# First FFN product of an fp32 attention and FFN kernel computed by Strassen's seven block products, with weights streamed per batch

## The reference, cut to what matters

```python
attn = softmax(scale * q @ k.T + bias, masked) @ v         # 2 batches, 8 heads, 768 x 64; window of 96 keys + 8 global
x = attn laid out as [2, 768, 512]
h = x.transpose(0, 2, 1) @ U @ V;  u = x + h.transpose(0, 2, 1)
x = u + np.maximum(u @ w_ch1, 0.0) @ w_ch2                 # layer 1: 512 -> 2048 -> 512
mixed = real(fft over the 768 rows, then over the 512 columns of x);  u = x + mixed
un = (u - mean) / sqrt(var + 1e-6)
out = u + np.maximum(un @ w_ch1, 0.0) @ w_ch2              # layer 2, its own weights
```

## Time and profile before

| | us |
|---|---|
| median of 3 runs | 726.27 |
| lowest, highest | 722.5, 728.18 |
| profiled execution, its own time | 723.18 |
| its span in the trace | 721.4 |
| TensorE busy | 707.2 (98%) |
| VectorE, ScalarE, GpSimd busy | 268.1, 160.5, 122.4 |
| DMA | 37.09 MB, mean 51 GB/s |
| mean granted TensorE clock | 0.992 of full |

### The profile page before, as it was taken

How to read it: one execution, slowest core, us unless ns; L and a number is a source line. 1 busy time by engine, 2 the same in 40 slices (tenths; PEclk the granted TensorE clock), 3 DMA queues, 4 the chain that set the end, 5 groups by cost and what they waited for, 6 DMA issues and landing times.

```text
span 721.4 us, 9877 instructions
## 1 busy us (share of the span) xinstructions
PE 707.2 (98%) x3888; PEld 639.8 (89%) x3888; DVE 268.1 (37%) x671; ACT 160.5 (22%) x445; POOL 122.4 (17%) x77
## 2 busy tenths in 40 slices
PE   8899999999999999999999979999999999999998
PEld 6799999999999989999979869888999999989897
DVE  7466543453231221213526976245612121212212
ACT  4466543432111111111211212212211111111110
POOL 1633000000042482000002551000000850000000
PEclk9899999999999999999999999999999999999999
DMA  7663222000023131000000211000000310101011
GB/s 203 205 220 127 100 99 98 2 2 0 1 77 96 50 125 60 0 0 1 0 1 30 88 58 59 1 0 1 1 1 0 116 59 0 44 0 44 6 37 44
DMA packets 28499, 37.09 MB, mean 51 GB/s; under 512 B 2896, under 2 KB 19408, under 8 KB 28336
## 3 DMA queue, kind: packets, MB, share of 16 engines
q1 hardware_dynamic: 28464, 36.62, 15.6%
HBM read 36.61 MB, written 3.15 MB: 55 GB/s over the span
## 4 chain that ended last, share of the span: by engine, by line
PE 92%; DVE 5%; SPq 2%; DMA 1%; issue 0%; ACT 0%; DVEq 0%
PE hidP L609 12%; PE hidP L611 12%; PE yP L620 12%; PE yP L621 12%; PE yP L622 12%; PE hidP L610 12%; PE aP L545 4%; PE aP L519 4%; PE aP L532 2%; PE yP L545 1%; PE hidP L569 1%; PE yP L519 1%; DVE Y L1116 1%; DMA K<-k_win 1%; DVE UN L1133 1%; PE aP L653 1%
## 5 line engine op out<-in xcount | busy, mean ns | idle before, releaser
L1028 DVE SCALAR_TENSOR_TENSOR hidL<-hidP,hidH 128x384 fp32r<-128x384 f32 x128 | 71.2, 556 | 324.1 <-ACT hidH L795 324.1
L609 PE MATMUL hidP<-UTH,WH 128*128 (+1 forms) x512 | 173.8, 339 | 0.0
L611 PE MATMUL hidP<-UTH,WL 128*128 (+1 forms) x512 | 172.4, 337 | 0.0
L610 PE MATMUL hidP<-UTL,WH 128*128 (+1 forms) x512 | 171.8, 336 | 0.0
L620 PE MATMUL yP<-WH,hidH 128*128 128x512 f32 x384 | 152.2, 396 | 0.0
L795 ACT ACTIVATE hidH<-hidP 128x384 fp32r<-128x384 f32 x128 | 62.9, 491 | 401.5 <-PE hidP L611 401.5
L622 PE MATMUL yP<-WH,hidL 128*128 128x512 f32 x384 | 151.9, 396 | 0.0
L621 PE MATMUL yP<-WL,hidH 128*128 128x512 f32 x384 | 151.6, 395 | 0.0
L609 PEld LDWEIGHTS hidP<-UTH,WH 128*128 128x128 f32 x512 | 96.3, 188 | 5.0 <-issue 1.2
L610 PEld LDWEIGHTS hidP<-UTL,WH 128*128 128x128 f32 x512 | 96.2, 188 | 3.6
L611 PEld LDWEIGHTS hidP<-UTH,WL 128*128 128x128 f32 x512 | 96.1, 188 | 0.0
(11 more groups left out here) (177 smaller groups left out, 563.5 us busy)
## 6 DMA issues: line engine op xcount, KB each, us to landing
w_stage<-w_in SPq DMA_DIRECT2D x32, 256.0 KB, 2.7
w_stage<-w_out SPq DMA_DIRECT2D x32, 256.0 KB, 3.0
V<-v_win SPq DMA_DIRECT2D x8, 704.0 KB, 7.0
K<-k_win SPq DMA_DIRECT2D x8, 644.0 KB, 5.6
Q<-q_t SPq DMA_DIRECT2D x16, 192.0 KB, 3.4
Y<-x_scratch SPq DMA_DIRECT2D x8, 384.0 KB
out<-Y SPq DMA_DIRECT2D x12, 256.0 KB, 2.0
CSraw<-seq_dft SPq DMA_DIRECT2D x1, 1348.0 KB, 7.0
```

The costliest lines, as they stand in the source:

```text
L609: nc.tensor.matmul(hidP[f % 2][:, 0:BLK], wh, rh, start=k == 0, stop=False)
L610: nc.tensor.matmul(hidP[f % 2][:, 0:BLK], wh, rl, start=False, stop=False)
L611: mm = nc.tensor.matmul(hidP[f % 2][:, 0:BLK], wl, rh, start=False, stop=k == KD - 1)
L1028: nc.vector.scalar_tensor_tensor(hidL[:, f % 2, :], hidP[f % 2][:, 0:BLK], 0.0, hi32(hidH[:, f % 2, :]), ALU.max, ALU.subtract).then_inc(s ...
```

## The change

The hidden layer is computed by Strassen's method in Winograd's form. A round takes two hidden tiles (256 units, rows of the block matrix A) and a whole batch of 768 tokens (two columns of blocks B of 384), with the 512 model rows in two halves: seven products of 2 x 3 matmuls of 384 columns each take the place of 8 x 2 x 3. 2 layers x 2 batches x 8 pairs of hidden tiles are 32 rounds (`ROUNDS`). The order on TensorE in a round is `ITEMS`; P is a product of this round, L a token tile (6 matmuls of 512 columns) of the second FFN product of the round before.

- POOL makes the sums of the weight blocks (`w_sums`: 4 of 128 x 256) and low parts (`w_lo`: 1792 columns, `o_lo`: 1024); ACT makes the high parts (`w_hi`, `o_hi`). Weights are loaded for every round, so twice per layer.
- POOL makes the sums of the token blocks (`u_sums`), ACT and DVE split all seven factors (`first_split` in slots 15, 21, 27 and 32 for the first batch, `split` between the items of two rounds for the other three).
- In a round ACT copies P1 and P5 out, DVE makes P1 + P6, adds it to P5 and makes the third sum, TensorE adds P2, P7, P3 and P4 on top.
- The second product has two banks in place of three, and DVE adds each into Y once per round: 192 adds in place of 48.
- Attention and its pieces are filled in behind every second item; the Fourier steps are spread 2.5 items apart, each batch starting one round after its last tile.
- Turned halves are kept in fp32 (RAW), so piece 3 is one fp32 transpose for a tile in place of two matmuls, and "turn" leaves only a copy on ACT.
- `pair(1)` is issued ahead of the branch and of the first weights; `w_load(1)` stands behind `pair(3)`.

```diff
+ITEMS = ("P1", "P5", "L0", "P6", "L1", "P2", "L2", "L3", "P7", "L4", "L5", "P3", "P4")
+FACTORS = {"P1": (A11, B11), "P2": (A12, B21), "P3": (S4, B22), "P4": (A22, T4), "P5": (S1, T1), "P6": (S2, T2), "P7": (S3, T3)}
+        BANKS = {"P1": Xb, "P2": Xb, "P5": Zb, "P3": Zb, "P6": Yb, "P7": Yb, "P4": Yb}
...
+            pair(1)
             beyond = all_keys(sp)
...
+            w_load(0)
+            o_load(0)
+            for n in range(2, 6):
                 pair(n)
                 final_x(n - 2)
+                if n == 3:
+                    w_load(1)
...
+            w_sums(0)
+            w_lo(0)
+            w_sums(1)
+            for k in range(KD):
+                u_sums(0, k)
+            for g in range(ROUNDS):
+                if g + 1 < ROUNDS:
+                    w_lo(g + 1)
+                o_lo(g)
+                if g + 2 < ROUNDS:
+                    w_sums(g + 2)
+                if g + 2 in CHANGES:
+                    for k in range(KD):
+                        u_sums(CHANGES.index(g + 2) + 1, k)
...
+                for k in range(KF):
+                    nc.tensor.matmul(bank, wh, uh, start=first and k == 0, stop=False, skip_group_check=True)
+                    nc.tensor.matmul(bank, wh, ul, start=False, stop=False, skip_group_check=True)
+                    mm = nc.tensor.matmul(bank, wl, uh, start=False, stop=k == KF - 1, skip_group_check=True)
...
+                if k < KF:
+                    nc.scalar.copy(UCH[:, B11, m, :], RAW[:, m, 0:BLK])
+                    act.wait_ge(s_tadd, k + 1)
+                    nc.scalar.copy(UCH[:, T1, m, :], TT[:, 0, m, :]).then_inc(s_uch, 1)
...
+                elif item == "P2":
+                    act.wait_ge(s_prod, made)
...
+                    if g > 0:
+                        act.wait_ge(s_y, TILES_OUT * (g - 1) + HT)
+                    relu(0, 0, Xb)
...
+            def tile_done(h, t):
+                dve.wait_ge(s_y, TILES_OUT * h + t + 1)
...
+                y = Y[:, NT * (h // FPAIRS % B) + t, :]
+                nc.vector.tensor_tensor(y, yP[t % 2][:, :], y, ALU.add).then_inc(s_yadd, 1)
```

More of the change, by code:

```diff
@@ L472, in nothing, with w_sums @@
-        def nothing(slot):
-            pass
+            def w_sums(g):
+                pool.wait_ge(s_wload, 64 * (g + 1))
+                if g > 0:
+                    pool.wait_ge(s_wl, 4 * g)
+                a21, a11, a12, a22, s1, s2, s3, s4 = (w_stage[:, u, :, :] for u in range(8))
+                nc.gpsimd.tensor_tensor(s1, a21, a22, ALU.add).then_inc(s_wadd, 1)
+                nc.gpsimd.tensor_tensor(s3, a11, a21, ALU.subtract).then_inc(s_wadd, 1)
+                pool.wait_ge(s_wadd, 4 * g + 1)
+                nc.gpsimd.tensor_tensor(s2, s1, a11, ALU.subtract).then_inc(s_wadd, 1)
+                pool.wait_ge(s_wadd, 4 * g + 3)
+                nc.gpsimd.tensor_tensor(s4, a12, s2, ALU.subtract).then_inc(s_wadd, 1)
@@ L582, in mix @@
                 else:
[L584 to L586 removed]
+                    pe.wait_ge(s_raw, 2 * pair + 2)
                     for t in range(HT):
[L588 to L590 removed]
+                        mm = nc.tensor.transpose(bank[:, P * t:P * t + P], RAW[:, k, BLK + P * t:BLK + P * t + P], identf[:, :])
                 mm.then_inc(s_piece, 1)
@@ new lines, in out_tile @@
+            def out_tile(h, t):
+                n = TILES_OUT * h + t
+                if t == 0:
+                    pe.wait_ge(s_hidl, 4 * (h + 1))
+                    pe.wait_ge(s_ol, 2 * (h + 1))
+                if n == 0:
+                    pe.wait_ge(s_ttr, 2 * STEPS)
+                elif n == 1:
+                    pe.wait_ge(*evacuated(STEPS - 1))
+                else:
+                    pe.wait_ge(s_yadd, n - 1)
+                bank = yP[t % 2]
+                for f in range(2):
+                    hh, hl = hidH[:, f, P * t:P * t + P], hidL[:, f, P * t:P * t + P]
+                    nc.tensor.matmul(bank[:, :], hh, WOH[:, h % 2, f, :], start=f == 0, stop=False)
+                    nc.tensor.matmul(bank[:, :], hh, WOL[:, h % 2, f, :], start=False, stop=False)
+                    mm = nc.tensor.matmul(bank[:, :], hl, WOH[:, h % 2, f, :], start=False, stop=f == 1)
+                mm.then_inc(s_y, 1)
@@ L787, in attention_slot, with split @@
+            def split(c, name):
+                j, op = PRODUCTS.index(name), FACTORS[name][1]
+                act.wait_ge(s_prod, len(PRODUCTS) * (CHANGES[c] - 1) + j + 1)
+                if j == 0:
+                    act.wait_ge(s_tadd, 2 * KD * (c + 2))
+                nc.scalar.copy(UCH[:, op, :, :], factor(op)).then_inc(s_uch, 1)
             def attention_slot(slot):
                 attention(slot)
-                for piece in pieces(slot):
-                    mix(*piece)
-            def ffn_block(g, fill=nothing, slot0=0):
-                def relu(f):
-                    act.wait_ge(s_hid, SEG * g + f + 1)
-                    nc.scalar.activation(hidH[:, f % 2, :], hidP[f % 2][:, 0:BLK], ACT.Relu).then_inc(s_hidh, 1)
-                relu(0)
-                for f in range(SEG):
-                    if f + 1 < SEG:
-                        relu(f + 1)
-                    fill(slot0 + 2 * f)
-                    fill(slot0 + 2 * f + 1)
+                for n in pieces(slot):
+                    mix(n)
+                if split_slot(slot) is not None:
+                    first_split(split_slot(slot))
+                if slot == 14:
+                    w_hi(0, 0)
+                    w_hi(0, 1)
@@ L821, in fourier @@
                     act.wait_ge(s_t, n + 1)
-                    c = S * b + HALF * part
+                    c = HALF * part
+                    if m == 0 and part == 0:
+                        act.wait_ge(s_ucl, splits(b + 1))
                     if m == KF:
```

669 lines of the change are left out of this document (397 added, 272 removed).

## The result

The changed kernel takes 742.95 us (median of 4 runs, 742.39 to 743.27), beside 727.22 us for the kernel before on the same chip: a ratio of 1.023, 95% interval 1.019 to 1.027. The forecast was 722, 0.6% faster. The time lies inside the range given (698 to 744), but near its slow end: a gain was forecast and a loss came.

The account below looks back on a forecast made before the run. TensorE, busy 98% of the span, was taken as the bound. The terms summed to -3.3 us: 719.9 on the profiled execution, 723.0 with 3.1 added for the median, stated as 722; range 698 to 744.

Parts of the forecast that it names:

- Factors of three batches: Two rounds per change: DVE's seven more low parts, two at places with 0.5 us of slack; +4.5 us (0 to 9).
- slot 15: First batch's splits: ACT's casts delay a copy, then ACT waits for POOL's sums behind a weight load; +12.5 us (5 to 14).
- products, bare rounds: FFN: 192 fewer first-product matmuls, -33.6 us; a round without filler takes 15.7 us and stalls nowhere, by 0.46 us.
- start, K: Slot 6: the earlier `pair(1)` removes the 2.84 us wait for K and the low clock; -5.0 us.
- FFN begins: Terms before the FFN: -5.0 start, +12.5 slot 15, +3.5 (1 to 6) splits at slots 21, 27, 32, half of piece 3's -2.7.
- attention between items: Rounds 0 to 6: attention's waits now stand behind ACT's wait for L5; +2 us (0 to 8).
- Fourier, both batches: Fourier stages: bursts and DVE waiting out POOL, 14 us first batch, 7 second; 21 against 7 before, +14 (0 to 26).
- last round: End of the kernel: no P1 and P5 stand ahead of L0; 1.5 us more.
- covers that hold: Rival: slot 15's load lands early (5 us), Fourier bursts cost 0, splits 3; about 695 us, range 693 to 710, chance 0.25.
- A bare round short of slack: Rival: 0.5 us more at the L2 to L4 place costs 32 rounds up to 0.7 each; +22, 744 us, chance 0.08.
- DVE becomes the bound by POOL: Rival, Fourier rounds: 38 DVE operations per batch each lose 1.0 us; 16 to 20 us on top, 740, chance 0.14.
- The Strassen saving: Rival, FFN products: no saving, since matmuls are bound by weight loads and not columns; 755 us, chance 0.01.

Follow-up runs that it names:

- experiment 2: Changed kernel without POOL's 24 later token sums and ACT's wait for them, T1 to T4's splits reading a plain block instead: 729.93 us, ratio 1.005.
- experiment 3: Changed kernel with the splits of plain blocks first, without a wait for the sums, and those of the sums from item 7 on: 736.38 us.
- after: The changed kernel as it was made, against the kernel before: 742.95 us, ratio 1.023.
- experiments 4 and 7: Changed kernel with, in 4, slot 15's token sums ahead of weight sums: 735.75 us; in 7, CSL in three instructions and the dim table earlier: 742.19 us.
- experiment 6: Kernel before with only the second pair's loads issued ahead of the branch and first weight tiles: 723.30 us, ratio 0.997.
- experiment 11: Changed kernel with POOL's weight sums and low parts 1 column long in rounds 9 to 13 and 17 to 21: 734.36 us, ratio 1.013.

## Why the prediction was wrong

The step that failed is "Factors of three batches": "two of them fall on places with 0.5 us of slack: 1.5 us x 3 = +4.5 us (0 to 9)". The three changes cost 21.6 us. I had counted DVE's seven low parts and their places, and had not walked the queue of their source: that ACT's first split waits for the last of eight sums on POOL, which POOL begins only as the round begins, and which instructions of ACT and DVE stand behind that wait. I had done exactly this for slot 15, where the same semaphore is waited for, and not for the three places where it recurs. The 21.6 us come apart like this:

- 3.3 us are what the term had counted, DVE's low parts: they are what is left in experiment 2, without the sums and the wait, with every split there. For these +4.5 was not far off.
- 13.0 us, 4.3 a change, are the sums and the wait for them, for which the term had nothing. Experiment 2 takes both out; experiment 3 keeps the sums, changes the order alone and gets 2.8 of the 4.3 back.
- 5.3 us are the clash of a split with CSL in rounds 7 and 8, with its lower clock, which the prediction didn't have either. It happened in after and not in the kernels of experiments 4 and 7; but their rounds 7 to 9 take 66.2 and 64.3 us together, where those of after take 66.1. So without it the kernel would have gained 0 to 2 us.

The bound of 9 was one of load and not of order, and so no bound.

Term by term, from the trace of after:

| term | forecast, us | measured, us |
|---|---|---|
| products, bare rounds | -33.6, 15.7 a round | 15.64 a round, no wait |
| start, K | -5.0 | step 13's product 5.1 earlier, with 1.4 of the next term in it: -6.5 |
| slot 15 | +12.5 | 1.38 + 9.48 of waits, some 2 for 3.62 us of work at clock 0.50: 12.7 |
| FFN begins (-5.0, +12.5, +3.5 and half of piece 3) | +9.7 | +9.2, good to some 3 |
| attention between items | +2 (0 to 8) | waits in rounds 0 to 6: 6.1 |
| factors of three batches | +4.5 (0 to 9) | +21.6 |
| Fourier, both batches | 21 | waits 10.1 and 7.5, work at a lower clock 3.2: 20.8 |
| last round | +1.5 | 1.17 |

From the beginning of the FFN on: -33.6 for the products, -1.4 for the other half of piece 3, 6.1, 21.6, 20.8 less the 7 that the Fourier stages cost before, and 1.2. With the 9.2 at its beginning that makes +16.9; the span grew by 19.9. For the other 3 us I have no row.

- **Right in mechanism and size:** the bare rounds, the wait for K (gone in after; the step alone gave 2.0 us in the kernel before, experiment 6), the wait at slot 17 with its place and its 7 to 10 us, the fold held by CDL in round 9 (waits of 0.90 and 3.15 us, where 1.5 and 4 had been said), the last round. The Fourier sum is right in size, 13.3 us for the first batch and 7.5 for the second where 14 and 7 had been said, but by luck in part: of the 17.6 us of waits 4.1 are the hold in round 9, 4.5 go when POOL's work goes (experiment 11), and 8.3 stand in rounds 13, 14, 21 and 22 and aren't POOL's doing. The 3.2 us are those by which TensorE's work in rounds 9 to 14 exceeds that in 17 to 22, at a clock of 0.97.
- **Right, mis-sized:** attention between the items, by 4 us, inside its bounds. POOL's instructions are 0.74, 1.02 and 1.28 us at 256, 384 and 512 columns, where I had scaled 2.46 us for 1024 down to 0.62, 0.9 and 1.2.
- **The rivals:** covers that hold is refuted by the rows of slot 17. A bare round short of slack is refuted by 15.64 us. That DVE becomes the bound by POOL is right in that its adds wait out POOL's instructions (experiment 11) and wrong in its price: some 5 us for both stages in all and not 16 to 20 on top. The price doesn't add up in itself either: 8 + 7 + 5 is 20 for a batch, 7 of which the forecast had, so 26 for two. The Strassen saving is there.
- That 743 was inside the range is luck: the range reached up there only for two other rivals, and neither is what happened; the chance for slower, 0.26, was too low because the one step that made it slower was not among them.
